# Recurrent attention and two feed-forward layers: reordered first tiles, last columns kept by VectorE, scores beside turn

## The chip, the cores and the metric

The kernel runs on one NeuronCore of a Trainium2 chip. The metric is the device time of one execution in microseconds (us). It was 442.21 us before the change, the median of three runs (441.96 to 442.27). Engines are TensorE (PE in the profile, PEld its weight loads), VectorE (DVE), ScalarE (ACT), GpSimd (POOL) and SyncE (SP), which here only issues DMAs.

## What is computed

Three layers, one after the other, in float32:

```python
for t in range(S):                       # B=2, H=8, S=768, D=40
    m_new = np.maximum(f_gate[:, :, t] + m, i_gate[:, :, t])
    f_stab = np.exp(f_gate[:, :, t] + m - m_new)
    i_stab = np.exp(i_gate[:, :, t] - m_new)
    C = f_stab * C + i_stab * outer(v[t], k[t]);  n = f_stab * n + i_stab * k[t]
    y[t] = sigmoid(o_gate[t]) * (C @ q[t]) / np.maximum(np.abs(n @ q[t]), 1.0)
x = y as rows of 320, 1536 tokens
xn = x / sqrt(mean(x * x) + 1e-6) * rms_g
x2 = (silu(xn @ w_gate) * (xn @ w_val)) @ w_out      # 320 -> 1536 -> 320
h = x2 @ w_in;  out = np.maximum(0.01 * h, h) @ w_out2   # 320 -> 2048 -> 320
```

## The kernel before

The 1536 tokens are 12 tiles of 128. Tile n holds one stretch of 128 tokens of one batch entry; tiles 0 and 1 (FIRST = 2) begin the two sequences and have no earlier state.

**A tile of attention** goes through pieces, each a function per engine. `scores` (PE, L1055 on) multiplies keys and queries of the eight heads into two PSUM banks; ScalarE's `decay` makes the exponentials of the gates in `expo`, `keep_last` copies their last columns to `last_decay`; VectorE's `scores(n, z)` (L784) multiplies the exponentials by the scores in place, once for each half z of the heads. `from_state` (PE, L1085) reads the state, `within` (L1107) multiplies by the values, `update_state` (L1097) makes the state's increment from keys that GpSimd's `weigh_keys` has weighed by `last_decay`. VectorE's `denominator` and `finish` give the tile's rows, ScalarE's `square`, GpSimd's `inverse_rms` and ScalarE's `normalise` norm them. `turn` (PE, L1120) transposes them into PSUM, and from there ScalarE's `x_high` and VectorE's `x_low` write the two parts (high and low, in the fp32r format) of x: `x_hi`, `x_lo`, and `x_odd` for the last 64 features. from_state of tile n waits for x_low of tile n - 1 (`x_done`) and for both score products of tile n (`p_done`).

**The first feed-forward layer** runs in steps (`STEPS`, L29): 12 slices of 128 hidden features by groups of tokens. Steps 0 to 9 take tiles 0 and 1 (256 columns), steps 10 to 19 tiles 2 and 3 (256 columns), steps 20 and 21 the last two slices for all four tiles (512 columns), and from step 22 on a step has 512 columns. In step s, PE makes `gate(s)` and `value(s)`, eight matmuls each (L1140), then `out1` of an earlier step (L1179, L1183). ScalarE's `first1` (tanh), VectorE's `gated` (L884) and `hidden1` (L891) work on them, ScalarE's `high1` (L620) and VectorE's `low1` (L905) split the result. value(s) writes the one value bank, which low1(s - 1) still reads, so it waits for that:

```python
            def value(s):
                if s > 0:

                    pe.wait_ge(h_done, s)
```

**The order around the change** is written out by hand. The table `BESIDE` (L36) gives for each tile from 2 on the steps S, R, O, T beside which its scores, its from_state and update, its finish and its turning are done: tile 3 has (4, 5, 6, 7), tile 4 (7, 9, 10, 11). The engines' loops run over s and take `work = beside(s - 1)`, so that a piece of step 4 is issued in the turn of the loop of step 5. Eight tiles (3, 4, 6, 7, 8, 9, 10, 11) have their S at the T of an earlier tile: at steps 4, 7, 14, 17, 20, 23, 26 and 29. The tile finished (O) one step before the tile's T, as tile 2 at step 3, has its denominator and finish between gated and hidden1 of the loop's step 4.

Weight slices come by DMA into three buffers `raw`; ScalarE's `hi_weights` (L600, 1088 columns) writes the high part, GpSimd's `lo_weights` (L472, L474) the low one; the next DMA into a buffer waits for both. Tiles 0 and 1 are done ahead of step 0: their gates are scanned by VectorE (L746 to L763), their scores, within and update_state follow, then their turn. `first_x_high`, `x_low_main` and `x_low_odd` are VectorE's part of their x, `first_state` copies their states. The second feed-forward layer follows from step 46 on, and the change leaves it as it is.

## Time and profile before

| | before |
|---|---|
| median of 3 runs | 442.21 us (441.96 to 442.27) |
| the profiled execution's own time | 442.24 us |
| its span, first to last instruction | 440.5 us |
| PE busy | 428.9 us (97%) |
| PEld busy | 375.2 us (85%) |
| VectorE busy | 225.5 us (51%) |
| ScalarE busy | 193.8 us (44%) |
| GpSimd busy | 92.9 us (21%) |
| first matmul of gate(0) | 21.46 us |
| PE busy from 22 to 440 us | 412.3 of 418 us |

The span is the part of the execution's time between its first and last instruction. A row of a timeline has the start in us from the span's start, the length in us, the engine, the line, the operation, what it writes and reads, the shapes and how many instructions of the kind follow each other. In brackets stands how long the engine was idle before, and what ended that. Matmuls overlap in the pipeline, so the distance between starts tells what one costs, not its length.

### The profile page before, as it was taken

The page shows a single profiled execution, that of the slowest core. Times are in us where ns is not written, and L with a number is a line of the kernel's source. Part 1 is how long each engine was busy: PE and PEld are TensorE (multiplying, and loading weights), DVE is VectorE, ACT ScalarE, POOL GpSimd, SP SyncE. Part 2 cuts the span into 40 slices and gives each one's busy share as a digit, 9 for nine tenths or more (in the row PEclk, how much of TensorE's full clock was granted, in tenths as well). Part 3 has the DMA queues.
Part 4 walks back from the last instruction along what each step waited for, and adds up shares of the span by engine and source line. Part 5 has one row for each costly group of instructions (what it writes and reads, how often), then busy time and mean ns, then how long its engine had stood idle before and what let it go on. Part 6 is the DMA issues. An engine that isn't in the chain of part 4 may idle for free.

```text
span 440.5 us, 8225 instructions
## 1 busy us (share of the span) xinstructions
PE 428.9 (97%) x3237; PEld 375.2 (85%) x3237; DVE 225.5 (51%) x435; ACT 193.8 (44%) x431; POOL 92.9 (21%) x98
## 2 busy tenths in 40 slices
PE   6889999999999999999999999999999999999997
PEld 5779998999788888878888888989999999999996
DVE  7656756765466555456433335353333333533534
ACT  4777763655262535234333226553343343333332
POOL 1888862122111111002333003430000000000000
PEclk9999999999999999999999999999999999999999
DMA  6797634331203410001222101400000000100101
GB/s 199 266 309 236 217 110 125 125 111 50 88 18 107 128 49 0 1 1 33 65 67 65 34 1 44 121 1 1 0 1 0 1 1 1 37 25 0 61 0 60
DMA packets 10692, 30.42 MB, mean 69 GB/s; under 512 B 1296, under 2 KB 3264, under 8 KB 10656
## 3 DMA queue, kind: packets, MB, share of 16 engines
q1 hardware_dynamic: 10656, 29.92, 21.1%
q8 instruction: 25, 0.41, 0.4%
q14 instruction: 11, 0.09, 0.1%
HBM read 27.90 MB, written 2.01 MB: 68 GB/s over the span
## 4 chain that ended last, share of the span: by engine, by line
PE 81%; issue 6%; POOL 6%; ACT 3%; DVE 2%; DMA 1%; POOLq 0%; DVEq 0%; ACTq 0%
PE gate_ps L1140 22%; PE value_ps L1140 22%; PE out_ps L1217 9%; PE out_ps L1179 9%; PE turn_ps L1217 6%; POOL w_sb L472 4%; PE out_ps L1183 3%; PE c_ps L1217 3%; PE turn_ps L1107 2%; PE turn_ps L1068 1%; PE turn_ps L1085 1%; ACT expo L543 1%; POOL w_sb L474 1%; POOL expo L441 1%; DMA y_acc<-in_first_gates 1%
## 5 line engine op out<-in xcount | busy, mean ns | idle before, releaser
L1140 PE MATMUL gate_ps<-x_hi,w_sb 128*128 128x512 f32 (+1 forms) x280 | 68.3, 365 | 1.6 <-ACT x_hi L582 0.8
L1140 PE MATMUL value_ps<-x_hi,w_sb 128*128 128x512 f32 (+1 forms) x280 | 68.4, 366 | 1.3 <-DVE h_lo L905 1.3
L1140 PEld LDWEIGHTS gate_ps<-x_hi,w_sb 128*128 128x128 f32 x280 | 46.8, 188 | 10.2 <-issue 1.9
L1140 PEld LDWEIGHTS value_ps<-x_hi,w_sb 128*128 128x128 f32 x280 | 47.1, 188 | 8.7 <-DVE h_lo L905 1.9
L884 DVE SCALAR_TENSOR_TENSOR act_buf<-act_buf,gate_ps 128x512 f32<-128x512 f32 (+1 forms) x46 | 26.2, 569 | 48.0 <-ACT act_buf L606 47.9
L910 DVE TENSOR_TENSOR h_lo<-hid,h_hi 128x512 fp32r<-128x512 f32 x48 | 33.2, 693 | 33.7 <-ACT h_hi L625 33.7
L620 ACT ACTIVATE h_hi<-value_ps 128x512 fp32r<-128x512 f32 (+1 forms) x46 | 23.0, 501 | 59.7 <-DVE value_ps L891 59.5
L1179 PE MATMUL out_ps<-h_hi,w_sb 128*128 128x512 f32 (+1 forms) x184 | 48.2, 348 | 0.0
L625 ACT ACTIVATE h_hi<-hid 128x512 fp32r<-128x512 f32 x48 | 30.3, 632 | 37.6 <-DVE hid L898 36.6
L606 ACT ACTIVATE act_buf<-gate_ps 128x512 f32<-128x512 f32 (+1 forms) x46 | 23.1, 501 | 49.2 <-PE gate_ps L1140 49.1
L480 POOL TENSOR_TENSOR w_sb<-raw,w_sb 128x704 fp32r<-128x704 f32 x16 | 27.6, 1724 | 76.6 <-ACT w_sb L600 76.6
L1217 PE MATMUL out_ps<-w_sb,h_hi 128*128 128x320 f32 x192 | 43.0, 309 | 0.2 <-DVE h_lo L910 0.2
L1140 PE MATMUL gate_ps<-x_lo,w_sb 128*128 128x512 f32 (+1 forms) x140 | 39.1, 360 | 0.0
L1140 PE MATMUL gate_ps<-x_odd,w_sb 128*128 128x512 f32 (+1 forms) x140 | 38.9, 359 | 0.1
L1140 PE MATMUL value_ps<-x_lo,w_sb 128*128 128x512 f32 (+1 forms) x140 | 38.9, 359 | 0.0
L1140 PE MATMUL value_ps<-x_odd,w_sb 128*128 128x512 f32 (+1 forms) x140 | 38.8, 358 | 0.0
L891 DVE SCALAR_TENSOR_TENSOR value_ps<-act_buf,value_ps 128x512 f32<-128x512 f32 (+1 forms) x46 | 26.5, 577 | 21.7 <-PE value_ps L1140 21.4
L905 DVE TENSOR_TENSOR h_lo<-value_ps,h_hi 128x512 fp32r<-128x512 f32 (+1 forms) x46 | 26.5, 575 | 21.1 <-ACT h_hi L620 20.7
L1179 PEld LDWEIGHTS out_ps<-h_hi,w_sb 128*128 128x128 f32 x184 | 31.4, 188 | 3.9
L898 DVE SCALAR_TENSOR_TENSOR hid<-gate_ps,act_buf 128x512 f32<-128x512 f32 x24 | 16.6, 692 | 34.8 <-ACT act_buf L613 34.8
L1217 PEld LDWEIGHTS out_ps<-w_sb,h_hi 128*128 128x128 f32 x192 | 32.7, 188 | 1.8 <-DVE h_lo L910 0.6
L898 DVE SCALAR_TENSOR_TENSOR hid<-value_ps,act_buf 128x512 f32<-128x512 f32 x24 | 16.6, 691 | 30.3 <-ACT act_buf L613 30.3
(150 smaller groups left out, 795.9 us busy)
## 6 DMA issues: line engine op xcount, KB each, us to landing
raw<-in_w SPq DMA_DIRECT2D x12, 544.0 KB, 4.8
att_sb<-in_tok SPq DMA_DIRECT2D x12, 484.0 KB, 4.5
raw<-in_w SPq DMA_DIRECT2D x16, 352.0 KB, 3.0
expo<-decay_scratch SPq DMA_DIRECT2D x10, 512.0 KB, 5.4
att_sb<-in_qk SPq DMA_DIRECT2D x24, 160.0 KB
out_y<-y_acc SPq DMA_DIRECT2D x12, 160.0 KB, 1.9
consts_sb<-in_consts SPq DMA_DIRECT2D x1, 129.5 KB, 2.4
y_acc<-in_first_gates SPq DMA_DIRECT2D x1, 112.0 KB, 2.7
```

The costliest lines, as they stand in the source:

```text
L480: nc.gpsimd.tensor_tensor(w[:, W2RAW:W2], r, w[:, 0:W2RAW].bitcast(F32), ALU.subtract).then_inc(w_lo, 1)
L606: nc.scalar.activation(act_buf[:, s % RING, 0:n], gate_ps[:, 0:n], ACT.Tanh, scale=0.5)\
L620: nc.scalar.activation(h_hi[:, r, cols], value_ps[:, 0:width(s)], ACT.Copy).then_inc(hi_done, 1)
L625: nc.scalar.activation(h_hi[:, r, :], hid[:, r, :], ACT.Copy).then_inc(hi_done, 1)
L884: nc.vector.scalar_tensor_tensor(out=a, in0=a, scalar=1.0, in1=gate_ps[:, 0:n], op0=ALU.add, op1=ALU.mult).then_inc(gate_used, 1)
L891: nc.vector.scalar_tensor_tensor(out=value_ps[:, 0:n], in0=act_buf[:, s % 2, 0:n], scalar=0.5, in1=value_ps[:, 0:n], op0=ALU.mult, op1=ALU ...
L898: nc.vector.scalar_tensor_tensor(out=hid[:, r, :], in0=in_ps[r][:, :], scalar=0.01, in1=act_buf[:, r, :], op0=ALU.mult, op1=ALU.max)\
L905: nc.vector.tensor_tensor(h_lo[:, r, cols], value_ps[:, 0:width(s)], h_hi[:, r, cols].bitcast(F32), ALU.subtract).then_inc(h_done, 1)
L910: nc.vector.tensor_tensor(h_lo[:, r, :], hid[:, r, :], h_hi[:, r, :].bitcast(F32), ALU.subtract).then_inc(h_done, 1)
L1140: last = nc.tensor.matmul(ps[:, 0:n], lhs, rhs, start=(j == 0), stop=(j == len(xs) - 1))
L1179: nc.tensor.matmul(out_ps[k][:, cols], lhs, rhs[:, r, place], start=(f == 0 and t == 0 and j == 0), stop=(f == NF1 - 1 and j == 2))
L1217: ins = nc.tensor.matmul(y_ps(i, k)[:, 0:DM], lhs[:, r, tok], rhs, start=(f == 0 and j == 0), stop=(f == GF - 1 and j == 2))
```

## The change

**Tiles 0 and 1.** On PE, `update_state(1)` goes from ahead of the turns to behind them, right before gate(0); the small product of the later tables goes ahead of turn(0). The second 128 features of tile 1 are turned into another bank (`main_ps`), the last 64 features of both tiles side by side into the value bank, so that ScalarE and VectorE make `x_odd` of both at once, 256 columns wide. The high parts of tile 1 are shared: ScalarE takes the first 128 features, VectorE the second. gate(0) waits for the two high parts one by one. VectorE takes over the last columns of tiles 0 and 1 from ScalarE, as four copies of 128x4, each with a wait of VectorE for itself (`first_kept`) ahead of the score product; GpSimd's weigh_keys waits for them. The subtraction of the later tiles' input gates (16 rows, 640 columns) goes from GpSimd to VectorE, behind the score products.

**Weight conversions on ScalarE.** The third goes from behind the turning of the first tiles to between their two squares, the fourth from behind first1(0) to ahead of it, and the fifth, in step 1, from ahead of the exponentials and high1 to behind high1.

**Tiles 3, 4 and 6 to 11.** Where a step turns a tile and takes the next tile's scores (`joined`), PE takes the scores behind turn instead of ahead of gate, and VectorE's two score products go to the end of the step instead of around gated.

```diff
+        def joined(s):
+
+            return beside(s - 1)["S"] and beside(s - 1)["T"]
@@ gpsimd
             def weigh_keys(n):
-                pool.wait_ge(last_done, n + 1)
+                if n < FIRST:
+                    pool.wait_ge(first_kept, 2 * n + 2)
+                else:
+                    pool.wait_ge(last_done, n - FIRST + 1)
...
-            nc.gpsimd.tensor_tensor(ig[0:NG, rest], ig[0:NG, rest], stab[0:NG, rest], ALU.subtract).then_inc(a_done, 1)
@@ scalar
                 for z in range(2):
                     decay(n, z)
-                keep_last(n)
             ogate(0)
             ogate(1)
             hi_weights(0)
+            hi_weights(1)
             square(0)
-            hi_weights(1)
+            hi_weights(2)
             square(1)
...
-            hi_weights(2)
+            hi_weights(3)
             first1(0, width(0))
-            hi_weights(3)
...
-                weights_last = work["T"] or work["O"] and beside(s)["S"]
+                weights_last = work["T"] or beside(s)["S"]
@@ vector
-                dve.wait_ge(last_done, n + 1)
+                if n < FIRST:
+                    dve.wait_ge(decay_done, 2 * n + z + 1)
+                    w = expo[:, n, :].rearrange("p (h t) -> p h t", h=H)[:, z::2, P - 1:P]
+                    nc.vector.tensor_copy(last_decay[:, n, z::2].unsqueeze(2), w).then_inc(first_kept, 1)
+                    dve.wait_ge(first_kept, 2 * n + z + 1)
...
+            nc.vector.tensor_tensor(ig[0:NG, rest], ig[0:NG, rest], m, ALU.subtract).then_inc(a_done, 1)
             for n in range(FIRST):
                 denominator(n)
                 finish(n)
...
-                for n in work["S"]:
+                for n in work["S"] if not joined(s) else ():
                     scores(n, 0)
...
-                for n in work["S"] if not h_first(s) else ():
+                for n in work["S"] if not h_first(s) and not joined(s) else ():
                     scores(n, 1)
...
+                for n in work["S"] if joined(s) else ():
+                    scores(n, 0)
+                    scores(n, 1)
@@ tensor
-            for n in range(FIRST):
-                update_state(n)
-            turn(0)
+            update_state(0)
             pe.wait_ge(tab_done, 3)
             nc.tensor.matmul(later_last_ps, last_row_sb, a_tab[:, NG:], start=True, stop=True).then_inc(tab_ps, 1)
+            turn(0)
             turn(1)
+            update_state(1)
...
-                for n in work["S"]:
+                for n in work["S"] if not joined(s) else ():
                     scores(n)
...
                 for n in work["T"]:
                     turn(n)
+                for n in work["S"] if joined(s) else ():
+                    scores(n)
```

On TensorE around step 5, where tile 2 is turned and tile 3's scores are taken. Before (L1183 is the end of out1, L1068 the scores, L1140 gate and value, L1120 and L1121 turn; three more such pairs of L1068 stand behind the pair shown):

```order
L1183 MATMUL out_ps<-h_lo,w_sb 128x256
L1068 MATMUL turn_ps<-att_sb 128x128
L1068 MATMUL c_ps<-att_sb 128x128
L1140 MATMUL gate_ps<-x_hi,w_sb 128x256 x4
L1140 MATMUL gate_ps<-x_lo,w_sb 128x256 x2
L1140 MATMUL gate_ps<-x_odd,w_sb 128x256 x2
L1140 MATMUL value_ps<-x_hi,w_sb 128x256 x4
L1140 MATMUL value_ps<-x_lo,w_sb 128x256 x2
L1140 MATMUL value_ps<-x_odd,w_sb 128x256 x2
L1120 MATMUL turn_ps<-consts_sb,xn 128x128 x2
L1121 MATMUL turn_ps<-consts_sb,xn 64x128
L1179 MATMUL out_ps<-h_hi,w_sb 128x256 x2
```

With the change (L1216 is out1's end, L1173 gate and value, L1151 and L1154 turn, L1099 the scores, L1212 the next out1):

```order
L1216 MATMUL out_ps<-h_lo,w_sb 128x256
L1173 MATMUL gate_ps<-x_hi,w_sb 128x256 x4
L1173 MATMUL gate_ps<-x_lo,w_sb 128x256 x2
L1173 MATMUL gate_ps<-x_odd,w_sb 128x256 x2
L1173 MATMUL value_ps<-x_hi,w_sb 128x256 x4
L1173 MATMUL value_ps<-x_lo,w_sb 128x256 x2
L1173 MATMUL value_ps<-x_odd,w_sb 128x256 x2
L1151 MATMUL turn_ps<-consts_sb,xn 128x128 x2
L1154 MATMUL turn_ps<-consts_sb,xn 64x128
L1099 MATMUL turn_ps<-att_sb 128x128
L1099 MATMUL c_ps<-att_sb 128x128
L1212 MATMUL out_ps<-h_hi,w_sb 128x256 x2
```

Again three more pairs stand behind the pair shown. The eight rows of the scores went from ahead of gate to behind turn.

On VectorE in the same step, from low1 of step 4 on (h_lo), before (L784 the score products, L860 and L871 x_low, L905 low1):

```order
L905 TENSOR_TENSOR h_lo<-value_ps,h_hi 128x256
L784 TENSOR_TENSOR expo<-expo,turn_ps 128x4x128
L884 SCALAR_TENSOR_TENSOR act_buf<-act_buf,gate_ps 128x256
L784 TENSOR_TENSOR expo<-expo,c_ps 128x4x128
L891 SCALAR_TENSOR_TENSOR value_ps<-act_buf,value_ps 128x256
L860 SCALAR_TENSOR_TENSOR x_lo<-turn_ps,consts_sb,x_hi 128x128 x2
L871 SCALAR_TENSOR_TENSOR x_odd<-turn_ps,consts_sb,x_odd 64x128
L905 TENSOR_TENSOR h_lo<-value_ps,h_hi 128x256
L884 SCALAR_TENSOR_TENSOR act_buf<-act_buf,gate_ps 128x256
```

and with the change (L806 the score products, L882 and L899 x_low, L933 low1):

```order
L933 TENSOR_TENSOR h_lo<-value_ps,h_hi 128x256
L912 SCALAR_TENSOR_TENSOR act_buf<-act_buf,gate_ps 128x256
L919 SCALAR_TENSOR_TENSOR value_ps<-act_buf,value_ps 128x256
L882 SCALAR_TENSOR_TENSOR x_lo<-turn_ps,consts_sb,x_hi 128x128 x2
L899 SCALAR_TENSOR_TENSOR x_odd<-turn_ps,consts_sb,x_odd 64x128
L933 TENSOR_TENSOR h_lo<-value_ps,h_hi 128x256
L806 TENSOR_TENSOR expo<-expo,turn_ps 128x4x128
L806 TENSOR_TENSOR expo<-expo,c_ps 128x4x128
L912 SCALAR_TENSOR_TENSOR act_buf<-act_buf,gate_ps 128x256
```

Both score products went behind low1 of step 5.

On ScalarE in steps 0 and 1, from first1 of step 0 on, before (L606 first1, L600 a weight conversion, L543 exponentials, L552 last columns, L620 high1):

```order
L606 ACTIVATE act_buf<-gate_ps 128x256
L600 ACTIVATE w_sb<-raw 128x1088
L543 ACTIVATE expo<-expo,c_tab 128x128 x4
L620 ACTIVATE h_hi<-value_ps 128x256
L606 ACTIVATE act_buf<-gate_ps 128x256
L600 ACTIVATE w_sb<-raw 128x1088
L543 ACTIVATE expo<-expo,c_tab 128x128 x4
L552 ACTIVATE last_decay<-expo 128x8
L620 ACTIVATE h_hi<-value_ps 128x256
```

and with the change, from one row ahead of first1 on (L617 the conversion, L623 first1, L555, L563, L637 in the same roles):

```order
L617 ACTIVATE w_sb<-raw 128x1088
L623 ACTIVATE act_buf<-gate_ps 128x256
L555 ACTIVATE expo<-expo,c_tab 128x128 x4
L637 ACTIVATE h_hi<-value_ps 128x256
L623 ACTIVATE act_buf<-gate_ps 128x256
L555 ACTIVATE expo<-expo,c_tab 128x128 x4
L563 ACTIVATE last_decay<-expo 128x8
L637 ACTIVATE h_hi<-value_ps 128x256
L617 ACTIVATE w_sb<-raw 128x1088
```

The first conversion went ahead of first1, the second behind high1 of step 1.

## Rows read from the trace of the kernel before

**Rows 1.** The page: busy times, and the granted clock in 40 slices.
```profile
PE 428.9 (97%) x3237; PEld 375.2 (85%) x3237; DVE 225.5 (51%) x435; ACT 193.8 (44%) x431; POOL 92.9 (21%) x98
...
PEclk9999999999999999999999999999999999999999
```

**Rows 2.** Timeline of TensorE, step 4's out1 to tile 3's from_state: start, length, instruction.
```profile
40.11 0.28 PE L1183 MATMUL out_ps<-h_lo,w_sb 128*128 128x256 f32 x1
...
41.41 0.74 PE L1140 MATMUL gate_ps<-x_hi,w_sb 128*128 128x256 f32 x4
...
42.46 0.63 PE L1140 MATMUL value_ps<-x_hi,w_sb 128*128 128x256 f32 x4
...
44.68 0.63 PE L1140 MATMUL gate_ps<-x_hi,w_sb 128*128 128x256 f32 x4
...
45.90 0.68 PE L1085 MATMUL turn_ps<-state,att_sb 40*64 40x41 f32 x32
```

**Rows 3.** Timeline of VectorE in the same stretch.
```profile
41.66 0.42 DVE L905 TENSOR_TENSOR h_lo<-value_ps,h_hi 128x256 fp32r<-128x256 f32 x1 [0.56 <-ACT h_hi L620]
...
43.73 0.68 DVE L784 TENSOR_TENSOR expo<-expo,c_ps 128x512 f32<-128x512 f32 x1
...
45.46 0.34 DVE L871 SCALAR_TENSOR_TENSOR x_odd<-turn_ps,consts_sb,x_odd 64x128 fp32r<-64x128 f32 x1
```

**Rows 4.** Timeline of TensorE: from_state of tiles 4 and 6.
```profile
61.17 0.68 PE L1085 MATMUL turn_ps<-state,att_sb 40*64 40x41 f32 x32
...
86.84 0.68 PE L1085 MATMUL turn_ps<-state,att_sb 40*64 40x41 f32 x32
```

**Rows 5.** Timeline of VectorE: low1 of steps 7, 14, 20 and 23.
```profile
54.13 0.42 DVE L905 TENSOR_TENSOR h_lo<-value_ps,h_hi 128x256 fp32r<-128x256 f32 x1 [0.56 <-ACT h_hi L620]
...
82.60 0.42 DVE L905 TENSOR_TENSOR h_lo<-value_ps,h_hi 128x256 fp32r<-128x256 f32 x1 [0.56 <-ACT h_hi L620]
...
108.65 0.69 DVE L905 TENSOR_TENSOR h_lo<-value_ps,h_hi 128x512 fp32r<-128x512 f32 x1 [0.67 <-ACT h_hi L620]
...
131.34 0.69 DVE L905 TENSOR_TENSOR h_lo<-value_ps,h_hi 128x512 fp32r<-128x512 f32 x1 [0.67 <-ACT h_hi L620]
```

**Rows 6.** Timeline of TensorE: last out1 ahead of tiles 8's and 9's scores.
```profile
108.53 0.28 PE L1183 MATMUL out_ps<-h_lo,w_sb 128*128 128x256 f32 x1
...
129.12 0.39 PE L1183 MATMUL out_ps<-h_lo,w_sb 128*128 128x512 f32 x1
```

**Rows 7.** Timeline of VectorE from the start to step 0.
```profile
7.45 0.81 DVE L761 TENSOR_TENSOR y_acc<-y_acc 16x640 f32<-16x640 f32 x1
...
12.71 0.69 DVE L784 TENSOR_TENSOR expo<-expo,value_ps 128x512 f32<-128x512 f32 x1 [0.91 <-ACT last_decay L552]
...
16.11 0.17 DVE L823 TENSOR_SCALAR den<-turn_ps 128x8 f32<-128x8 f32 x1 [0.67 <-PE turn_ps L1107]
...
22.25 0.34 DVE L871 SCALAR_TENSOR_TENSOR x_odd<-value_ps,consts_sb,x_odd 64x128 fp32r<-64x128 f32 x1
...
24.47 0.43 DVE L891 SCALAR_TENSOR_TENSOR value_ps<-act_buf,value_ps 128x256 f32<-128x256 f32 x1
```

**Rows 8.** Timeline of TensorE: value in steps 1 and 2.
```profile
26.51 0.74 PE L1140 MATMUL value_ps<-x_hi,w_sb 128*128 128x256 f32 x4 [0.74 <-DVE h_lo L905]
...
30.52 0.72 PE L1140 MATMUL value_ps<-x_hi,w_sb 128*128 128x256 f32 x4 [0.56 <-DVE h_lo L905]
```

**Rows 9.** Timeline of ScalarE in steps 0 to 2.
```profile
24.46 1.27 ACT L543 ACTIVATE expo<-expo,c_tab 128x128 f32<-128x128 f32 x4
...
27.21 1.11 ACT L600 ACTIVATE w_sb<-raw 128x1088 fp32r<-128x1088 f32 x1 [0.94 <-DMA raw<-in_w]
...
29.64 0.36 ACT L620 ACTIVATE h_hi<-value_ps 128x256 fp32r<-128x256 f32 x1
```

**Rows 10.** Timeline of TensorE: two turned pieces of 128 columns, of tile 1 and of tile 2.
```profile
19.86 0.63 PE L1120 MATMUL out_ps<-consts_sb,xn 128*128 128x128 f32 x2
...
43.40 0.38 PE L1120 MATMUL turn_ps<-consts_sb,xn 128*128 128x128 f32 x2
```

More of the change, by code:

```diff
@@ L259, in build @@
         t_done = sem("t_done")
-        first_xhi = sem("first_xhi")
-        xhi_part = sem("xhi_part")
+        t_part = sem("t_part")
+        xhi_part = [sem(f"xhi_part{k}") for k in range(2)]
         xlo_part = sem("xlo_part")
@@ L576, in x_high @@
             def x_high(n):
-                act.wait_ge(t_done, n + 1)
+                tok = slice(n * P, (n + 1) * P)
                 if n == 1:
                     act.wait_ge(consts_in, 16)
-                tok = slice(n * P, (n + 1) * P)
-                for k in range(2):
-                    ins = nc.scalar.activation(x_hi[:, k, tok], turned_ps(n)[:, k * P:(k + 1) * P], ACT.Copy,
-                                               scale=rms_sb[:, k:k + 1])
-                if n < FIRST:
-                    ins.then_inc(xhi_part, 1)
-                nc.scalar.activation(x_odd[0:ODD, tok], odd_ps(n), ACT.Copy,
-                                     scale=rms_sb[0:ODD, 2:3]).then_inc(xhi_done, 1)
+                    act.wait_ge(t_part, 1)
+                    nc.scalar.activation(x_hi[:, 0, tok], main_ps(n, 0), ACT.Copy, scale=rms_sb[:, 0:1])\
+                        .then_inc(xhi_part[0], 1)
+                act.wait_ge(t_done, n + 1)
+                for k in range(2) if n > 1 else ():
+                    nc.scalar.activation(x_hi[:, k, tok], main_ps(n, k), ACT.Copy, scale=rms_sb[:, k:k + 1])
+                if n == 1:
+                    nc.scalar.activation(x_odd[0:ODD, FIRST_TOK], first_odd_ps, ACT.Copy,
+                                         scale=rms_sb[0:ODD, 2:3]).then_inc(xhi_done, 1)
+                else:
+                    nc.scalar.activation(x_odd[0:ODD, tok], odd_ps(n), ACT.Copy,
+                                         scale=rms_sb[0:ODD, 2:3]).then_inc(xhi_done, 1)
             def hi_weights(i):
@@ L748, in _ @@
             nc.vector.tensor_tensor(fg[:, 1:P], fg[:, 1:P], stab[:, 1:P], ALU.subtract)
-            nc.vector.memset(fg[:, 0:1], 0.0)
-            then(nc.vector.tensor_tensor(ig[:, now], ig[:, now], stab[:, now], ALU.subtract))
+            then(nc.vector.memset(fg[:, 0:1], 0.0))
             nc.vector.tensor_tensor_scan(acum[:, now], restart[:, now], fg[:, now], 0.0, ALU.mult, ALU.add)\
                 .then_inc(a_done, 1)
+            then(nc.vector.tensor_tensor(ig[:, now], ig[:, now], stab[:, now], ALU.subtract))
             dve.wait_ge(a_done, 1)
@@ L844, in first_x_high @@
                 for k in range(2):
-                    ins = nc.vector.tensor_scalar(x_hi[:, k, 0:P], turned_ps(0)[:, k * P:(k + 1) * P],
-                                                  rms_sb[:, k:k + 1], None, ALU.mult)
-                ins.then_inc(xhi_part, 1)
-                nc.vector.tensor_scalar(x_odd[0:ODD, 0:P], odd_ps(0), rms_sb[0:ODD, 2:3],
-                                        None, ALU.mult).then_inc(first_xhi, 1)
+                    nc.vector.tensor_scalar(x_hi[:, k, 0:P], main_ps(0, k), rms_sb[:, k:k + 1], None, ALU.mult)\
+                        .then_inc(xhi_part[k], 1)
+                dve.wait_ge(t_part, 2)
+                nc.vector.tensor_scalar(x_hi[:, 1, P:2 * P], main_ps(1, 1), rms_sb[:, 1:2], None, ALU.mult)\
+                    .then_inc(xhi_part[1], 1)
             def x_low_main(n):
-                if n == 1:
-                    dve.wait_ge(xhi_part, FIRST)
-                elif n:
+                if n < FIRST:
+                    for k in range(2):
+                        dve.wait_ge(xhi_part[k], n + 1)
+                else:
                     dve.wait_ge(xhi_done, n)
-                else:
-                    dve.wait_ge(first_xhi, 1)
                 tok = slice(n * P, (n + 1) * P)
@@ L865, in x_low_main, with first_low_odd @@
                     ins.then_inc(xlo_part, 1)
+            def first_low_odd():
+                dve.wait_ge(xhi_done, 1)
+                nc.vector.scalar_tensor_tensor(
+                    out=x_odd[ODD:P, FIRST_TOK], in0=first_odd_ps, scalar=rms_sb[0:ODD, 2:3],
+                    in1=x_odd[0:ODD, FIRST_TOK].bitcast(F32), op0=ALU.mult, op1=ALU.subtract).then_inc(x_done, FIRST)
             def x_low_odd(n):
-                if n:
-                    dve.wait_ge(xhi_done, n)
+                dve.wait_ge(xhi_done, n)
                 tok = slice(n * P, (n + 1) * P)
@@ L1132, in in_product @@
                 for j, (lhs, rhs) in enumerate(xs):
-                    if tiles and j == 0:
-                        pe.wait_ge(xhi_part, tiles)
+                    if tiles and j in (0, 2):
+                        pe.wait_ge(xhi_part[j // 2], tiles)
                     elif tiles and j == 4:
@@ L1241, in _ @@
             table(later_c_ps, ig, 1, SEQ_TILES)
-            for n in range(FIRST):
-                update_state(n)
-            turn(0)
+            update_state(0)
             pe.wait_ge(tab_done, 3)
             nc.tensor.matmul(later_last_ps, last_row_sb, a_tab[:, NG:], start=True, stop=True).then_inc(tab_ps, 1)
+            turn(0)
             turn(1)
+            update_state(1)
             gate(0)
```

24 lines of the change are left out of this document (15 added, 9 removed).

## The prediction

> **What bounds the kernel now.** I read the page first, then the timelines of TensorE, VectorE and ScalarE side by side around each place that the change touches. The page says where a microsecond counts: TensorE is busy for 428.9 of 440.5 us and no other arithmetic engine for more than 51%, with the granted clock at its upper level, 2.4 GHz, in all slices [rows 1]. From about 60 us on, it has practically no gap. So work that leaves another engine gains nothing; what counts is a gap that closes or opens on TensorE. A gap opened there is never made up.
>
> The reader should see two things in the timeline around step 5 [rows 2, 3]. First, tile 3's scores lie between the last out1 of step 4 (next slot 40.11 + 0.12 = 40.23) and gate of step 5 (41.41): they take 1.18 us. Second, value of step 5 has to wait for low1 of step 4, which VectorE ends at 41.66 + 0.42 = 42.08; value starts at 42.46. Only 0.4 us of margin is left, and the scores are what makes it. A step in which VectorE also finishes a tile (denominator, finish) and ScalarE also squares has its low1 late. Such a step stands just ahead of each of the eight steps that turn a tile and take the next one's scores.
>
> **The joined scores, narrow steps.** Tiles 3, 4, 6 and 7 are joined in steps 5, 8, 15 and 18, of 256 columns. Count tile 3. A product of 256 columns (gate or value, eight matmuls) takes 42.46 - 41.41 = 1.05 us with the restart after the scores, 0.11 of which is that restart (0.74 against 0.63 for its first four), so 0.94 plain [rows 2]. Without the scores ahead, gate starts at 40.23 and ends at 41.17. Value needs low1, which nothing in the change makes earlier: 42.08 + 0.06 = 42.14. **TensorE waits 0.97 us**, and value starts only 0.32 earlier than before.
>
> The scores now follow turn, and their products on VectorE follow x_low and low1 of the same step. From value's start to the end of x_low it was 45.46 + 0.34 - 42.46 = 3.34 us [rows 2, 3], a chain through turn, x_high and x_low that stays; I add 0.1 for value's restart after a wait. So x_low ends at 45.58. Then low1 (0.03 + 0.34 until the next can start), two score products (0.60 + 0.68 by the row of 0.68) and 0.1 to TensorE: from_state can start at 47.3. TensorE would be ready at 42.14 + 0.1 + 2.22 (value to the next gate [rows 2]) + 1.1 for the scores + 0.94 = 46.5. It waits again, 0.8 us, and starts 1.4 later than the 45.90 of before. Behind that wait stand within, update_state and value; on VectorE the next gated stands behind the products, but its reader, a gate two products on, comes later. I take **+1.35**.
>
> Tile 6 gives the same by its own rows: low1 ends at 82.60 + 0.42 = 83.02, value at 83.08, from_state 3.44 + 0.37 + 1.28 + 0.1 = 5.2 later at 88.27, against 86.84 [rows 4, 5]: +1.4. Tile 7 repeats this pattern. Three tiles: **+4.1**. Tile 4's from_state comes one step later, so its products are hidden. Value of step 8 can start at 54.13 + 0.42 + 0.06 = 54.61, 0.32 earlier than before by the same margin, and the scores (1.18, less the 0.1 of a restart) lie after it: **+0.75** on the 61.17 [rows 4, 5].
>
> **The joined scores, wide steps.** Products of 512 columns take 2 x 0.94 = 1.9 us. Tile 8: last out1 at 108.53 + 0.12, gate until 110.5; low1 has ended at 108.65 + 0.69 = 109.3. No wait. Tile 9: last out1 at 129.12 + 0.23, gate until 131.2; low1 (late, since the chunk's x2 lies there) ends at 131.34 + 0.69 = 132.03. TensorE waits 0.85: **+0.75** net [rows 5, 6]. Tiles 10 and 11 go as tile 8, whose products have another 1.9 us of out1 and 1.9 of gate as cover. There the move gives a little: the change of tile shape between out1 and scores, scores and gate, and turn and out1 becomes one fewer. The row prices a restart at 0.11 [rows 2]: **-0.1** each, three times. The Trainium skill (TensorEngine Tiling (Array Packing), Key Properties) says that changing the tiling mode drains the engine; by that rule turn (64 columns) to scores (40 rows) is a change too, and the gain stays the one restart.
>
> **The start.** ScalarE loses two copies of last columns; VectorE gets four of 128x4 and the 16x640 subtraction from GpSimd. The nearest rows are 0.17 for 8 columns (0.20 with its wait) and 0.81 for the same subtraction [rows 7]. Four copies are 0.8 us, in place of the 0.91 that VectorE sat waiting for ScalarE; behind each copy's wait stands a score product, and behind that TensorE's within. GpSimd only gets free earlier, and its first weight slice waits for ScalarE's conversion as before; the DMA queue's order is unchanged. The subtraction goes ahead of the first denominator, where 0.67 was idle before the second: 0.15 is left over. ScalarE converts a third weight slice (1.1 us) between the two squares, so the second starts some 0.2 late. Against this VectorE drops one x_odd piece ahead of the last that gate 0 waits for (ended 22.25 + 0.34), worth 0.3, and one update_state moves into TensorE's gap before gate 0, which was there anyway. **0**, with -0.3 to +0.6 as bounds.
>
> **Steps 1 and 2.** Value of step 1 waited 0.74 and value of step 2 waited 0.56 for low1 [rows 8]. In step 0 ScalarE took a weight conversion between first1 and the exponentials that started at 24.46, and only then high1; it is now ahead of first1. The exponentials start 1 us earlier, and high1 then follows hidden1 (24.47 + 0.43 = 24.90) by itself: value 1 at about 25.9, -0.65. In step 1 the conversion of 27.21 (which sat 0.94 for its DMA first) moves behind high1, which had started at 29.64 [rows 9]; value 2 is then bound by the work ahead of it, 1.05 + 1.18 + 1.05 after value 1: 29.2 in place of 30.52. **-1.35** in all. Bounds: 0 if the wait only changes its name, -1.9 if the start gains too.
>
> **The sum.** 4.1 + 0.75 + 0.75 - 0.3 - 1.35 = +3.95, say +4.0. The profiled execution took 442.24 us for a span of 440.5, and the median of the runs is 442.21, the same: **446.2 us**. A measurement of this kernel can tell about 0.2% (0.9 us) from nothing.
>
> **Rivals.**
> A. The cover is not needed (7%): faster. This needs low1 of the steps ahead of the joined ones to end 0.9 us earlier against TensorE than the rows show, as the conversions moved out of ScalarE's queue might bring. Then nothing is lost, and -1.35 - 0.8 gives 440.1. Against it: steps 14 and 17 have no conversion in them, and low1 of step 14 is just as late. It decides from 0.6 us of relief per joined step on.
> B. Only the first wait is real (12%): x_low and the products run closer than I chained them, so tiles 3, 6 and 7 cost 0.75 like tile 4. 5 x 0.75 - 0.3 - 1.35 = +2.1: 444.3.
> C. Steps 1 and 2 give nothing back (15%), since the raw slice's DMA or first_state on VectorE takes over the wait: 447.5.
> D. Slower clock (6%). Two turned pieces take 0.63 in tile 1 and 0.38 in tile 2 [rows 10]: the early one runs at about half the rate, though the page prints full clock. If the sparser work before gate 0 makes that last longer, the three products of steps 0 and 1 (0.94 each) take up to 2.8 more, partly inside waits: 447.7. The Trainium skill (TensorE: Matmul & The Clock Gate, Part 1) says that idle resets the clock to 1.2 GHz and sustained work raises it; by that rule a gap of 1 us later on costs no more than itself, or much more, and no row here shows such a gap.
> E. As forecast (60%).
>
> **How the numbers follow.** The range takes in B and, above, C and D together with 0.6 from the start: 443.6 to 448.2. Faster holds A (0.07). Same, within 0.9 us of 442.2, needs B with a start better than its bound or half of A: 0.04. Slower: 0.89.
>
> **What would show it.** Right: TensorE waits of some 0.9 us on value for VectorE's h_lo, five of them; waits on from_state for VectorE's expo, three of 0.6 to 0.9; the two waits of rows 8 gone or below 0.2; from_state of tile 3 near 45.9 + 1.4 - 1.35 = 45.9; after 200 us all work 4 us late. Wrong: low1 ending before gate does in steps 4, 7, 14, 17, or the gaps closing again in the second layer.

## The result, and the profile after

The changed kernel takes **446.3 us** (median of 4 runs, 445.47 to 446.37) against 442.24 us for the kernel before in the same session (4 runs, 441.96 to 442.61). The ratio is 1.0088, 95% interval 1.0073 to 1.0103: slower by 0.9%, more than the 0.2% that can be told. The forecast was 446.2. The profiled execution took 446.29 us for a span of 444.6 us, 4.1 more than the 440.5 of before.

From the page of the changed kernel: busy times with their share of the span, and the granted clock in 40 slices.

```profile
PE 430.0 (97%) x3237; PEld 376.0 (85%) x3237; DVE 226.6 (51%) x439; ACT 193.0 (43%) x428; POOL 90.9 (20%) x97
...
PEclk9899999999999999999999999999999999999999
```

TensorE does the same 3237 matmuls in 430.0 us in place of 428.9 [rows 1], and the span grew by 4.1. So the loss is mostly gaps. The waits of TensorE in the changed kernel name them (us in total, times, longest):

```profile
PE value_ps L1173 <- DVE h_lo L933: 4.3, 7, 0.9
...
PE turn_ps L1116 <- DVE expo L806: 1.5, 3, 0.5
PE out_ps L1277 <- DVE c_tab L787: 0.9, 1, 0.9
```

Seven waits of value and three of from_state (L1116) are there. The 0.9 for `c_tab` lies ahead of gate(0). The timeline of TensorE around step 5 of the changed kernel, columns as in [rows 2], shows the first of each:

```profile
36.90 0.74 PE L1173 MATMUL value_ps<-x_hi,w_sb 128*128 128x256 f32 x4 [0.26 <-DVE h_lo L933]
...
38.80 0.28 PE L1216 MATMUL out_ps<-h_lo,w_sb 128*128 128x256 f32 x1
38.92 0.64 PE L1173 MATMUL gate_ps<-x_hi,w_sb 128*128 128x256 f32 x4
...
40.95 0.74 PE L1173 MATMUL value_ps<-x_hi,w_sb 128*128 128x256 f32 x4 [0.91 <-DVE h_lo L933]
...
44.58 0.64 PE L1173 MATMUL gate_ps<-x_hi,w_sb 128*128 128x256 f32 x4
...
46.20 0.68 PE L1116 MATMUL turn_ps<-state,att_sb 40*64 40x41 f32 x32 [0.50 <-DVE expo L806]
```

and the timeline of VectorE in the same stretch, against [rows 3]:

```profile
40.47 0.42 DVE L933 TENSOR_TENSOR h_lo<-value_ps,h_hi 128x256 fp32r<-128x256 f32 x1 [0.56 <-ACT h_hi L637]
...
44.06 0.34 DVE L899 SCALAR_TENSOR_TENSOR x_odd<-turn_ps,consts_sb,x_odd 64x128 fp32r<-64x128 f32 x1
44.44 0.42 DVE L933 TENSOR_TENSOR h_lo<-value_ps,h_hi 128x256 fp32r<-128x256 f32 x1
44.78 0.68 DVE L806 TENSOR_TENSOR expo<-expo,turn_ps 128x512 f32<-128x512 f32 x1
45.38 0.68 DVE L806 TENSOR_TENSOR expo<-expo,c_ps 128x512 f32<-128x512 f32 x1
```

Gate of step 5 now starts 0.12 us after the last out1, with no scores between. low1 ends at 40.47 + 0.42 = 40.89 and value starts at 40.95: TensorE has stood for 0.91 us. In place of the 1.18 of scores there is a hole. Further on, x_low ends at 44.40, then low1 and the two products follow in a row to 46.06, and from_state starts at 46.20 after a second hole of 0.50. VectorE itself is not full here: it idles 1.30 us before gated of step 5. It is late in order, not in load.

The other narrow joined tiles repeat this; these rows of the timeline of TensorE are value of steps 8 and 15, from_state of tile 6, value of step 18, from_state of tile 7, value of step 24, to be read against [rows 4, 6]:

```profile
54.92 0.74 PE L1173 MATMUL value_ps<-x_hi,w_sb 128*128 128x256 f32 x4 [0.74 <-DVE h_lo L933]
...
84.44 0.74 PE L1173 MATMUL value_ps<-x_hi,w_sb 128*128 128x256 f32 x4 [0.73 <-DVE h_lo L933]
...
89.68 0.68 PE L1116 MATMUL turn_ps<-state,att_sb 40*64 40x41 f32 x32 [0.51 <-DVE expo L806]
...
98.39 0.74 PE L1173 MATMUL value_ps<-x_hi,w_sb 128*128 128x256 f32 x4 [0.72 <-DVE h_lo L933]
...
103.64 0.68 PE L1116 MATMUL turn_ps<-state,att_sb 40*64 40x41 f32 x32 [0.51 <-DVE expo L806]
...
136.21 1.21 PE L1173 MATMUL value_ps<-x_hi,w_sb 128*128 128x512 f32 x4 [0.79 <-DVE h_lo L933]
```

**Ledger.** Below is the start of the same piece of TensorE's work in the two profiled executions, and what the step cost. "fs" is from_state.

| piece | before | after | difference | this step |
|---|---|---|---|---|
| gate(0) | 21.46 | 20.56 | -0.90 | -0.90 |
| value(1) | 26.51 | 24.99 | -1.52 | -0.62 |
| value(2) | 30.52 | 28.28 | -2.24 | -0.72 |
| value(4) | 38.35 | 36.90 | -1.45 | +0.79 |
| fs of tile 3 | 45.90 | 46.20 | +0.30 | +1.75 |
| fs of tile 4 | 61.17 | 62.47 | +1.30 | +1.00 |
| fs of tile 6 | 86.84 | 89.68 | +2.84 | +1.54 |
| fs of tile 7 | 99.13 | 103.64 | +4.51 | +1.67 |
| fs of tile 8 | 118.10 | 122.23 | +4.13 | -0.38 |
| fs of tile 9 | 138.42 | 143.55 | +5.13 | +1.00 |
| fs of tile 11 | 179.06 | 183.88 | +4.82 | -0.31 |
| value(69), near the end | 430.25 | 434.33 | +4.08 | -0.74 |

The start and steps 0 to 2 gave back 2.24 us, a late weight slice took 0.79, the joined tiles took 6.27, and 0.7 came back slowly in the wide steps. The row of tile 11 holds tiles 10 and 11.

The +0.79 at value(4) was not expected. This is the timeline of ScalarE in the changed kernel, steps 0 to 5:

```profile
22.90 1.27 ACT L555 ACTIVATE expo<-expo,c_tab 128x128 f32<-128x128 f32 x4
24.09 0.38 ACT L637 ACTIVATE h_hi<-value_ps 128x256 fp32r<-128x256 f32 x1
...
27.98 1.11 ACT L617 ACTIVATE w_sb<-raw 128x1088 fp32r<-128x1088 f32 x1 [0.82 <-DMA raw<-in_w]
...
35.01 1.11 ACT L617 ACTIVATE w_sb<-raw 128x1088 fp32r<-128x1088 f32 x1 [2.80 <-DMA raw<-in_w]
36.02 0.37 ACT L637 ACTIVATE h_hi<-value_ps 128x256 fp32r<-128x256 f32 x1
```

The exponentials start at 22.90, and high1 at 24.09, against 24.46 and 29.64 (step 1) in [rows 9]: the conversions are out of the way. But the conversion at 35.01 sits 2.80 us for a weight slice that lands no sooner than before, and high1 of step 3 stands behind it. Value(4) waits 0.26 and is 1.45 ahead in place of 2.24. When this slice lands differs from profile to profile, though. In the kernel with only tiles 8, 10 and 11 joined (below), which is the same up to here, ScalarE's timeline has it 0.87 earlier:

```profile
34.14 1.11 ACT L617 ACTIVATE w_sb<-raw 128x1088 fp32r<-128x1088 f32 x1 [2.30 <-DMA raw<-in_w]
```

There value(4) does not wait and is 2.26 ahead of before. In two more such kernels the conversion starts at 34.89 (not joined) and 33.49 (products ahead of low1), again with no wait at value(4); with the products late only it starts at 34.62, and value(4), 2.6 ahead one step earlier, waits 0.56. So the loss of 0.79 belongs to this profiled execution rather than to every one of this kernel.

### The profile page after: what moved, and what is told of

It reads as the page before. It is cut to its first block, busy times and chain, and to the rows that moved or that the text cites. A ratio compares the mean times of both kernels' runs of the same rounds, so it can differ in the third digit from the quotient of the medians.

```text
span 444.6 us, 8229 instructions
## 1 busy us (share of the span) xinstructions
PE 430.0 (97%) x3237; PEld 376.0 (85%) x3237; DVE 226.6 (51%) x439; ACT 193.0 (43%) x428; POOL 90.9 (20%) x97
## 4 chain that ended last, share of the span: by engine, by line
PE 75%; issue 7%; DVE 6%; POOL 4%; DMA 4%; ACT 3%; SPq 0%; DVEq 0%; POOLq 0%; ACTq 0%
PE value_ps L1173 21%; PE gate_ps L1173 20%; PE out_ps L1250 9%; PE out_ps L1212 8%; PE turn_ps L1250 6%; PE c_ps L1250 3%; PE out_ps L1216 3%; POOL w_sb L487 3%; DMA raw<-in_w 2%; PE turn_ps L1138 2%; PE turn_ps L1099 1%; DMA att_sb<-in_tok 1%; PE turn_ps L1116 1%; ACT expo L555 1%; DVE value_ps L919 1%
## 5 line engine op out<-in xcount | busy, mean ns | idle before, releaser
L1173 PE MATMUL value_ps<-x_hi,w_sb 128*128 128x512 f32 (+1 forms) x280 | 69.0, 367 | 4.3 <-DVE h_lo L933 4.3
L1173 PE MATMUL gate_ps<-x_hi,w_sb 128*128 128x512 f32 (+1 forms) x280 | 67.9, 364 | 0.2
L1173 PEld LDWEIGHTS value_ps<-x_hi,w_sb 128*128 128x128 f32 x280 | 47.2, 188 | 12.8 <-DVE h_lo L933 5.9
L1173 PEld LDWEIGHTS gate_ps<-x_hi,w_sb 128*128 128x128 f32 x280 | 47.7, 191 | 7.4 <-DVE x_odd L899 0.5
L637 ACT ACTIVATE h_hi<-value_ps 128x512 fp32r<-128x512 f32 (+1 forms) x46 | 23.0, 501 | 58.9 <-DVE value_ps L919 58.6
L1212 PE MATMUL out_ps<-h_hi,w_sb 128*128 128x512 f32 (+1 forms) x184 | 48.3, 349 | 0.0
L623 ACT ACTIVATE act_buf<-gate_ps 128x512 f32<-128x512 f32 (+1 forms) x46 | 23.0, 500 | 53.6 <-PE gate_ps L1173 53.5
L1173 PE MATMUL gate_ps<-x_lo,w_sb 128*128 128x512 f32 (+1 forms) x140 | 39.2, 361 | 0.0
L1173 PE MATMUL gate_ps<-x_odd,w_sb 128*128 128x512 f32 (+1 forms) x140 | 39.0, 360 | 0.0
L1173 PE MATMUL value_ps<-x_lo,w_sb 128*128 128x512 f32 (+1 forms) x140 | 39.0, 360 | 0.0
L1173 PE MATMUL value_ps<-x_odd,w_sb 128*128 128x512 f32 (+1 forms) x140 | 38.8, 359 | 0.0
L933 DVE TENSOR_TENSOR h_lo<-value_ps,h_hi 128x512 fp32r<-128x512 f32 (+1 forms) x46 | 26.5, 575 | 20.9 <-ACT h_hi L637 20.6
L1212 PEld LDWEIGHTS out_ps<-h_hi,w_sb 128*128 128x128 f32 x184 | 31.6, 189 | 4.8
```

Of the source, the lines that this page charges most:

```text
L623: nc.scalar.activation(act_buf[:, s % RING, 0:n], gate_ps[:, 0:n], ACT.Tanh, scale=0.5)\
L637: nc.scalar.activation(h_hi[:, r, cols], value_ps[:, 0:width(s)], ACT.Copy).then_inc(hi_done, 1)
L933: nc.vector.tensor_tensor(h_lo[:, r, cols], value_ps[:, 0:width(s)], h_hi[:, r, cols].bitcast(F32), ALU.subtract).then_inc(h_done, 1)
L1173: last = nc.tensor.matmul(ps[:, 0:n], lhs, rhs, start=(j == 0), stop=(j == len(xs) - 1))
L1212: nc.tensor.matmul(out_ps[k][:, cols], lhs, rhs[:, r, place], start=(f == 0 and t == 0 and j == 0), stop=(f == NF1 - 1 and j == 2))
```

## The experiments

Each kernel ran in five rounds against the kernel before on the same chip; the ratio is to that. The kernel before took 442.1 us in the session of the first four kernels and 441.97 us in that of the last four. The diffs are to the changed kernel, save where the text says otherwise.

### Without the joined scores

```diff
         def joined(s):
-            return beside(s - 1)["S"] and beside(s - 1)["T"]
+            return False
```

> The changed kernel with joined always false: the eight tiles' scores and products go back to their old places, the rest of the change stays. Theory (the joined scores take away TensorE's cover in the narrow steps): summed over the eight joined tiles, from_state is 5.9 us later in the changed kernel than in the one before, so this gives 440.4 us (440.0 to 440.9), the waits on value for h_lo in steps 5, 8, 15, 18 and 24 and those on from_state for expo are gone, and the gain of steps 0 to 2 is kept. Rival (the loss is in the start: the clock at half between 19 and 22 us, and the later conversions): it stays near 446, or at least above 443.

Measured: 439.95 us (439.57 to 440.21), ratio 0.9948 (0.9934 to 0.9961). All but one of value's waits are gone, as the waits of TensorE in this kernel say:

```profile
PE value_ps L1173 <- DVE h_lo L933: 0.4, 1, 0.4
```

The waits of from_state are gone too. The time is 0.05 us below the range that was expected. The joined scores cost 446.3 - 439.95 = 6.35 us (6.1 between the spans of the two profiles), and the rest of the change is worth 2.15. The change is two changes of opposite sign; this half of it beats the kernel before.

### The joined scores alone

The kernel before, with `joined` and the five places that use it put in, three on VectorE and the two on TensorE that are shown:

```diff
+        def joined(s):
+            return beside(s - 1)["S"] and beside(s - 1)["T"]
...
-                for n in work["S"]:
+                for n in work["S"] if not joined(s) else ():
...
+                for n in work["S"] if joined(s) else ():
+                    scores(n)
```

> The kernel before with only the scores joined to turn, on TensorE and on VectorE. Theory: 442.2 + 5.9 = 448.1 us (447.3 to 448.6), five waits on value of 0.7 to 0.9 and three on from_state of about 0.5. Rival (the loss is in the start): near 442.2.

Measured: 448.01 us (447.72 to 448.06), ratio 1.0131 (1.0115 to 1.0146), +5.9. The waits of TensorE in this kernel:

```profile
PE value_ps L1147 <- DVE h_lo L909: 4.1, 5, 1.0
...
PE turn_ps L1092 <- DVE expo L788: 1.6, 3, 0.5
```

Five waits of value and three of from_state, with none from the start mixed in: the pattern of the prediction by itself. Seen from both sides, the joined scores cost 5.9 (added to before) and 6.35 (taken from the changed kernel). The start and the conversions give 2.15 without them and 448.01 - 446.3 = 1.7 with them.

### Joined only where the cover is to spare

```diff
         def joined(s):
-            return beside(s - 1)["S"] and beside(s - 1)["T"]
+            return beside(s - 1)["T"] and [n for n in beside(s - 1)["S"] if n in (8, 10, 11)]
```

> The changed kernel with only tiles 8, 10 and 11 joined, where the step has 512 columns and low1 is early enough. Theory: each gives one restart of TensorE, 0.1 to 0.4 us: 439.8 us (439.5 to 440.3), below the run without any joined tile by 0.3 to 0.7. Rival (putting scores right behind turn costs TensorE a further change of tile shape): not below that run, or up to 0.3 above it.

Measured: 439.81 us (438.96 to 440.02), ratio 0.9949 (0.9935 to 0.9962). Its median is 0.14 us below the kernel without joined scores, less than the runs scatter and less than the 0.3 that was expected at least, so the times alone do not settle it against the rival. In the two traces, tile 8 gains 0.43 and tiles 10 and 11 gain 0.05 each; the rest of the difference between the two profiles, 0.75, lies ahead of value(1), where the clock went differently (below). So no loss in these three tiles, and a gain in the traces that the medians don't resolve. These are the two best versions found, about 0.5% faster than the kernel before.

### Products ahead of low1

One part of the second hole is low1 standing ahead of the products on VectorE. Here the products go ahead of low1 in all joined steps but step 8. (`x_first` marks the steps whose low1 stands behind x_low; in these seven the next step's from_state needs the products.)

```diff
+                for n in work["S"] if joined(s) and x_first else ():
+                    scores(n, 0)
+                    scores(n, 1)
...
-                for n in work["S"] if joined(s) else ():
+                for n in work["S"] if joined(s) and not x_first else ():
```

> The changed kernel, with VectorE's two score products ahead of low1 of the same step instead of behind it (steps 5, 15 and 18 and the wide ones; step 8 as it is). Theory (from_state waits for the chain x_low, low1, products): from_state of tiles 3, 6 and 7 comes 0.37 us sooner each, so 445.2 us (444.9 to 445.6), with the value waits unchanged at about 0.9 and 0.7. Rival (from_state waits for TensorE's own scores or for x_low): unchanged at 446.3.

Measured: 445.01 us (444.37 to 445.57), ratio 1.0064 (1.005 to 1.0078). Waits of TensorE on from_state in this kernel:

```profile
PE turn_ps L1119 <- DVE expo L806: 0.5, 3, 0.2
```

Each of the three goes from 0.50 to 0.17 or 0.18, about the 0.34 that low1 takes on VectorE. Three times 0.33 is 1.0 of the 1.3 us between the medians; another 0.2 is there at value(5) already (40.72 against 40.95). The chain from value through x_low and the products to from_state is what sets those tiles, link by link.

### The conversions alone

The kernel before, with ScalarE's new order of conversions and nothing else:

```diff
             hi_weights(0)
-            square(0)
             hi_weights(1)
+            square(0)
+            hi_weights(2)
             square(1)
...
-            hi_weights(2)
+            hi_weights(3)
             first1(0, width(0))
-            hi_weights(3)
...
-                weights_last = work["T"] or work["O"] and beside(s)["S"]
+                weights_last = work["T"] or beside(s)["S"]
```

> The kernel before with only ScalarE's weight conversions in their new order. Theory (the waits of value for low1 in steps 1 and 2 came from conversions in ScalarE's queue): value of step 1 comes 0.65 us and value of step 2 1.35 us earlier, and 440.9 us results (440.5 to 441.5). Rival (the first tiles' new order is what pays): 442.2 or above, since the second square is late.

Measured: 441.47 us (440.58 to 441.76, 12 runs), ratio 0.9983 (0.9973 to 0.9992). A gain of 0.5 us, at the weak end of what was expected. Its profiled execution (440.8 us) is one of the better runs: there value(1) is 0.84 and value(2) 1.57 earlier, both of the waits of [rows 8] are gone, and 1.4 is kept to the end. The median of the runs keeps only a third of that; what the other executions do differently is not shown.

### The start alone

The kernel without joined scores, with the conversions back in their old order (the reverse of the diff above).

> The changed kernel without joined tiles and with the conversions in their old order: only the first tiles' part is left. Theory: gate of step 0 starts some 0.9 us sooner, but gated of step 0 still waits for VectorE's copies of the states and high1 for the exponentials, so 441.5 us (440.8 to 442.2), with the waits on value in steps 1 and 2 still there. Rival (the start carries all of the gain, the conversions nothing): 440.0.

Measured: 441.96 us (441.36 to 443.85, 12 runs), ratio 1.0001 (0.9989 to 1.0013): nothing. Its profile says why. gate(0) starts 0.98 earlier, and then the waits of TensorE have this:

```profile
PE value_ps L1173 <- DVE h_lo L933: 1.7, 2, 0.9
```

Value(1) waits 0.91 and value(2) 0.76, more than the 0.74 and 0.56 of [rows 8]. The head start is waited away behind ScalarE's conversions, and value(2), at 30.14, is 0.38 ahead, from_state of tile 6 0.07 behind. The clock was at half rate through gate(0) and value(0) in this profile (four matmuls 1.22 and 1.05 long), but it was so in that of the kernel without joined scores too, whose value(2) is at 28.93. So by the medians the start alone gives 0, the conversions 0.5 and both together 2.15, more than the sum by more than the intervals allow. One half of an explanation is in this profile: while the conversions stand where they did, the lead of the start is waited away. The other half is not shown. At value(69), near the end, the profile of the conversions alone is 1.43 ahead of before, that of the start alone 0.69 and that of both 2.00, which is about the sum.

### The late weight slice out of high1's way

The kernel with tiles 8, 10 and 11 joined, and the conversion of step 3 put behind high1 too:

```diff
-                weights_last = work["T"] or beside(s)["S"]
+                weights_last = work["T"] or beside(s)["S"] or s == 3
```

> The changed kernel with only tiles 8, 10 and 11 joined, and besides with the weight conversion of step 3 behind high1 instead of ahead of it. In the changed kernel's profile that conversion waited 2.8 us for its DMA and high1 of step 3 behind it, which made value of step 4 wait 0.26 us. Theory: 439.5 us (439.2 to 439.9), 0.3 below the run with the three tiles joined. Rival (the DMA's landing binds only in executions whose start went well, or high1 is late for another reason): the same as that run, 439.8.

Measured: 440.24 us (439.52 to 440.38), ratio 0.9952 (0.9937 to 0.9967). **A miss**: no gain over the 439.81 and the ratio of 0.9949 without the edit. The wait that the edit was to remove is one of the changed kernel's profile. In that of the kernel it was made to, the slice landed in time and value(4) did not wait, so there was nothing to win. Here value(4) doesn't wait either and is 1.83 ahead. But the conversion now lies at 35.62 for 1.1 us, ahead of the exponentials, and all of ScalarE's step behind it is late: on TensorE's timeline of this kernel the wait is there one step on.

```profile
36.52 0.64 PE L1173 MATMUL value_ps<-x_hi,w_sb 128*128 128x256 f32 x4
...
41.28 0.74 PE L1173 MATMUL value_ps<-x_hi,w_sb 128*128 128x256 f32 x4 [0.44 <-DVE h_lo L933]
```

Value(5) is 1.18 ahead of before, against 2.17 without the edit: value(4) to value(5) takes 4.76 in place of 4.20. The 1.1 us of conversion hold up ScalarE on either side of high1, and the step that finishes tile 2 has no room for them.

### Products late, scores where they were

TensorE takes the scores ahead of gate again, as before, and only VectorE's products stay late:

```diff
@@ tensor
-                for n in work["S"] if not joined(s) else ():
+                for n in work["S"]:
                     scores(n)
...
-                for n in work["S"] if joined(s) else ():
-                    scores(n)
```

> The changed kernel with TensorE's scores back ahead of gate in all eight tiles, while VectorE's two products stay at the end of the step. Theory: the waits of value for h_lo in steps 5, 8, 15, 18 and 24 vanish (the scores cover low1 again), those of from_state for expo grow, since value starts when it did and the chain behind it is 5.2 us against 3.4: tiles 3, 6 and 7 lose 1.6 each, so 444.7 us (444.0 to 445.2). Rival (all of the loss is the lost cover of low1): near 440.

Measured: 453.77 us (450.9 to 454.24, 6 runs), ratio 1.0237 (1.0208 to 1.0265). **A miss by 9 us**, and the slowest kernel of all. The timeline of TensorE in this kernel, value of step 5 and from_state of tile 3:

```profile
40.77 0.64 PE L1173 MATMUL value_ps<-x_hi,w_sb 128*128 128x256 f32 x4
...
45.92 0.68 PE L1116 MATMUL turn_ps<-state,att_sb 40*64 40x41 f32 x32 [1.80 <-DVE expo L806]
...
48.52 1.22 PE L1173 MATMUL value_ps<-x_hi,w_sb 128*128 128x256 f32 x4
```

The two holes of the changed kernel, 0.91 and 0.50, have become one of 1.80. Value(5) starts at 40.77 with no wait, and from_state at 45.92, 0.28 before the 46.20 of the changed kernel: x_low, low1 and the products on VectorE set it, wherever TensorE has the scores. Tiles 9, 10 and 11 wait another 0.3 each. The waits of 1.80 were foreseen. What wasn't is what comes after. Four matmuls of value take 1.22 us in place of 0.64, and the stretches of this kernel (us, then busy times of the engines with counts, then the granted clock, the DMA share and GB/s) say so:

```profile
40.00:47.00 7.00, 5.20 (x83) 4.97 (x84) 4.18 (x10) 5.18 (x11) 6.90 (x6) 1.00 0.83 266
47.00:50.50 3.50, 3.50 (x49) 3.42 (x46) 0.50 (x1) 0.00 (x0) 3.50 (x5) 0.51 0.54 159
50.50:60.00 9.50, 9.50 (x87) 9.25 (x87) 5.79 (x17) 8.13 (x23) 4.56 (x6) 1.00 0.54 192
91.40:98.30 6.90, 6.90 (x80) 6.77 (x72) 2.38 (x8) 1.74 (x6) 1.51 (x2) 0.51 0.01 2
98.30:108.50 10.20, 8.39 (x100) 7.97 (x100) 5.99 (x15) 5.24 (x17) 1.24 (x2) 1.00 0.43 134
108.50:115.30 6.80, 6.80 (x86) 6.55 (x79) 2.09 (x6) 1.39 (x5) 1.51 (x2) 0.50 0.01 2
```

Behind each of the three waits of 1.80 us (at 45.92, 90.89 and 108.11) the granted clock is at 0.50 or 0.51, that is 1.2 GHz, for 3.4, 6.8 and 6.8 us, while TensorE is busy all the time. Half of 17.0 us is 8.5 us lost. Together with 6.3 us of waits of from_state (three of 1.80, three of 0.3) that is 14.8; the span is 452.5 - 438.5 = 14.0 longer than that of the kernel without joined scores. The waits alone are less than half of it.

## Why the prediction was right

**The joined scores (forecast +4.1 + 0.75 + 0.75 - 0.3 = +5.3).** Measured +5.9 added alone, +6.35 taken out. The mechanism stood: five waits of value for low1 and three of from_state for the products, in the forecast tiles and no others, and rivals A and B fall. The waits of from_state, 0.50 and 0.51, were below the 0.6 to 0.9 given as a sign. A had value's waits unneeded; they are 0.72 to 0.91 long. B had the products close enough behind; they aren't. The terms, from the ledger:

- Tiles 6 and 7, +1.4 each forecast, +1.54 and +1.67 there. The chain on VectorE held: value's start to from_state was 89.68 - 84.44 = 5.24 at tile 6 (46.20 - 40.95 = 5.25 at tile 3), forecast 5.2, with the two products 1.28 long as forecast. The first wait reads 0.73 against 0.97, but the profile counts from the end of the last matmul and the forecast from where the next could start: from start to start the hole at value(15), whose gate starts at 82.59 and takes 0.96, is 84.44 - 83.55 = 0.89. The second, 0.5 in place of 0.8, was misjudged: TensorE's own work from value to the end of the next gate took 46.20 - 0.50 - 40.95 = 4.75 at tile 3, forecast 4.36. It costs nothing, since VectorE's chain ends later either way.
- Tile 3, +1.35 forecast, +1.75 there. The late weight slice shifted low1 of step 4 too: value(5) waited 0.91 where tiles 6 and 7 waited 0.73. In the kernel with the products ahead of low1, whose slice came in time, value(5) waited 0.72, as there.
- Tile 4 and tile 9, +0.75 each forecast, +1.0 each. **This is the term that was mis-sized**: the 0.1 of a restart was taken off, and the wait of value brings its own (four matmuls 0.74 long against 0.64). Behind turn the eight scores also push the next out1 back by 1.26 (1.29 from the last piece of turn to out1, against 0.03 before), where the forecast had 1.1.
- Tiles 8, 10 and 11, -0.1 each forecast. Tile 8 gave -0.38: in the kernel before, gate of step 22 started late behind x_low of the new chunk, and the scores now fill that stretch. Tiles 10 and 11 gave -0.16 each here, of which the kernel without joined scores has 0.10 as well, and -0.05 each in the experiment that joins 8, 10 and 11: half of what was said of one restart.

**Steps 1 and 2 (forecast -1.35).** Measured -0.62 and -0.72, -1.34 together, with value(1)'s wait down to 0.16 and value(2)'s gone. Rival C falls. The step was priced as the conversions' own. Their profile alone agrees (value(2) 1.57 earlier, 1.40 of it behind gate(0)), but their median gives only 0.5, and that difference is open.

**The start (forecast 0, bounds -0.3 to +0.6).** gate(0) came 0.90 earlier, outside the bound. The copies on VectorE cost what was said (0.16 each), and the pieces fit where it waited. The text took the gap ahead of gate(0) for a fixed one; its wait of 0.81 for x_hi is gone. By which of the start's edits was not tried apart. One of them the description of the change leaves out: in the gates' scan of tiles 0 and 1 a subtraction moved behind the second scan, and TensorE's wait for `y_acc` went from 1.1 to 0.8. In the two profiles without the start's edits gate(0) is at 21.24 and 21.29, so some 0.2 of the 0.90 is scatter. By itself this is worth nothing (the start alone is at 1.0001), so the 0 was right in the time and wrong in the trace.

**The weight slice (not in the forecast).** +0.79 at value(4). The text said that the raw slices come by an unchanged DMA queue, and looked no further than step 2. A lead gained on TensorE is kept only as far as the next thing that doesn't move with it. In this profile the slice was that thing and took 0.8; where it landed 0.87 earlier it took nothing.

**After 200 us** all was to be 4 us late, and is: +4.82 at tile 11 and +4.08 at the end. The drift of 0.7 between is not explained. Wide steps had a pitch of 5.49 us before and 5.44 after from step 34 to 45, with no wait in either. All ten profiles divide in the same way: 5.49 in the three without the start's edits (before, joined scores alone, conversions alone), 5.44 in the seven with them. So the drift goes with the start's edits and not with the joined scores.

So the total was right by 0.1 us, with misses of up to 1.0 in its terms: the start was 0.9 better, the slice 0.8 worse, the joined tiles 1.0 worse, the drift 0.7 better. The mechanism and the sign of the two large terms were right; that the misses cancelled to 0.1 was luck.

**Rival D (a slower clock, 6%)** came in part. The clock was at half rate from 19.0 to 22.4 us, and gate(0) took 22.42 - 20.56 = 1.86 us where it took 1.52 before; yet value(1) was 1.52 ahead. Such time can lie inside waits: in the profile of the joined scores alone the first four matmuls of gate(0), value(0) and gate(1) last 1.19, 1.05 and 1.05 us, the waits of [rows 8] are absent, and value(2) is still 0.32 ahead of before. The other half of D, a fall after a later gap, did not come: the clock held after the holes of 0.91 and 0.50 us. The experiment with the products late only shows its price.

## What to carry to other kernels

When an engine is busy 97% of the time, small work on it may be what covers another engine's latency: before moving it, add up who is to be ready when it is gone, and follow the chain to the next reader as well. A lead is worth only what the next arrival that doesn't move with it (a DMA, a conversion in a queue) leaves of it, and when that arrives may differ between executions: before an edit against a wait, see whether the kernel that is to be edited has that wait in its own profile. Two edits can be worth more together than the sum of their medians, so try them together too. Two short holes can be far cheaper than one long one, because a long one may cost the clock.
